# Attention with two heads stacked on partition halves as row tiles of TensorE, in a fused attention, ELU MLP and soft-MoE kernel

## What is computed

```python
def _attn_ref(q, k, v):
    B, H, S, D = q.shape                      # 4, 8, 1152, 64
    q_pool = q.reshape(B, H, S // 2, 2, D).mean(axis=3)
    scores = (1.0 / np.sqrt(D)) * np.matmul(q_pool, k.transpose(0, 1, 3, 2))
    scores = scores - np.max(scores, axis=-1, keepdims=True)
    attn = np.exp(scores)
    attn = attn / (np.sum(attn, axis=-1, keepdims=True) + 1e-09)
    return np.matmul(attn, v)

h = x @ w_in                                   # x: attention output, (2304, 512)
g = np.where(h > 0.0, h, np.exp(np.minimum(h, 0.0)) - 1.0)
x = g @ w_out
# soft MoE: logits = x @ phi; softmax over tokens gives the slots' inputs,
# two layers with a relu per expert, softmax over slots gives the outputs
```

## Time and profile before

| | |
|---|---|
| median of 3 runs | 1035.39 us (1034.98 to 1036.83) |
| profiled execution, span | 1034.5 us |
| granted TensorE clock, mean over the span | 0.979 of full speed |
| PE busy (matmul) | 959.7 us |
| DVE busy | 694.7 us |
| ACT busy | 499.0 us |
| POOL busy | 432.7 us |

### The profile page before, as it was taken

How to read it: one execution, slowest core, us unless ns; L and a number is a source line. 1 busy time by engine, 2 the same in 40 slices (tenths; PEclk the granted TensorE clock), 3 DMA queues, 4 the chain that set the end, 5 groups by cost and what they waited for, 6 DMA issues and landing times.

```text
span 1034.5 us, 17581 instructions
## 1 busy us (share of the span) xinstructions
PE 959.7 (93%) x6842; PEld 799.1 (77%) x6842; DVE 694.7 (67%) x1167; ACT 499.0 (48%) x1134; POOL 432.7 (42%) x155
## 2 busy tenths in 40 slices
PE   4799999999999999999979999999999999999795
PEld 2677667677667676767679999999999999999533
DVE  7769999999999999996577434444444444443423
ACT  3666666677666677665654323333323333232202
POOL 7887888988888888878900000000000000000000
PEclk9889999999999999999989999999999999999898
DMA  7621233322233332130061000020000000047995
GB/s 158 173 71 47 69 92 92 92 70 60 56 92 93 92 82 57 47 108 1 8 197 62 1 1 1 1 83 1 2 1 1 1 2 1 1 146 277 389 387 205
DMA packets 38946, 85.81 MB, mean 83 GB/s; under 512 B 3664, under 2 KB 11984, under 8 KB 38864
## 3 DMA queue, kind: packets, MB, share of 16 engines
q1 hardware_dynamic: 38864, 84.70, 27.1%
HBM read 79.97 MB, written 4.72 MB: 82 GB/s over the span
## 4 chain that ended last, share of the span: by engine, by line
PE 62%; DVE 32%; issue 3%; DMA 2%; ACT 1%; SPq 0%; DVEq 0%; ACTq 0%
DVE mx L921 8%; PE psum L530 7%; DVE kl L913 7%; PE psum L532 7%; PE psum L531 7%; PE psum L513 6%; PE psum L515 6%; PE psum L514 6%; DVE rinv L939 5%; DVE x L946 4%; PE psum L453 4%; DVE nm L932 3%; PE psum L454 3%; PE psum L421 3%; DVE q L903 2%
## 5 line engine op out<-in xcount | busy, mean ns | idle before, releaser
L1208 POOL TENSOR_TENSOR acc<-acc,pt 128x1152 f32<-128x1152 f32 x112 | 322.9, 2883 | 71.6 <-ACT pt L724 62.0
L724 ACT ACTIVATE pt<-psum 128x288 f32<-128x288 f32 x576 | 225.7, 412 | 153.4 <-PE psum L454 144.1
L921 DVE TENSOR_REDUCE mx<-psum 128x1 f32<-128x384 f32 x432 | 210.4, 546 | 30.8 <-PE psum L421 15.0
L453 PE MATMUL psum<-q,khh 128*128 128x288 f32 x576 | 181.0, 318 | 1.8 <-ACT pt L724 1.1
L454 PE MATMUL psum<-q,kl 66*128 66x288 f32 x576 | 170.8, 300 | 0.0
L530 PE MATMUL psum<-gh,W 128*128 128x288 f32 x512 | 158.4, 309 | 5.4 <-DVE gl L1002 5.4
L1080 DVE TENSOR_SCALAR g<-g 128x288 f32<-128x288 f32 x128 | 39.5, 309 | 175.1 <-ACT g L855 175.1
L532 PE MATMUL psum<-gh,W 128*128 128x288 f32 x512 | 151.6, 296 | 0.0
L513 PE MATMUL psum<-xh,W 128*128 128x288 f32 x512 | 151.6, 296 | 0.0
L514 PE MATMUL psum<-xl,W 128*128 128x288 f32 x512 | 151.4, 296 | 0.0
L531 PE MATMUL psum<-gl,W 128*128 128x288 f32 x512 | 151.2, 295 | 0.0
(11 more groups left out here) (113 smaller groups left out, 1393.5 us busy)
## 6 DMA issues: line engine op xcount, KB each, us to landing
ring<-in_w SPq DMA_DIRECT2D x32, 1024.0 KB, 7.5
kraw<-in_kT SPq DMA_DIRECT2D x64, 288.0 KB, 4.4
qraw<-in_qT SPq DMA_DIRECT2D x16, 576.0 KB, 5.7
vs<-in_v SPq DMA_DIRECT2D x16, 576.0 KB, 5.3
out<-ob SPq DMA_DIRECT2D x9, 512.0 KB, 4.9
wst<-in_w_in SPq DMA_DIRECT2D x16, 256.0 KB, 2.9
wst<-in_w_out SPq DMA_DIRECT2D x16, 256.0 KB, 3.6
sel<-in_selection SPq DMA_DIRECT2D x1, 96.0 KB, 8.3
```

The costliest lines, as they stand in the source:

```text
L453: mm(o, khh[:, p % NB, s, keys], q1[:, p % NB, a:a + HALF], start=True, stop=False)
L724: act.activation(pt[:, t % NPT, at:at + HALF], psum[:, T_BANKS[i % 3], 0:HALF], ACT.Exp, scale=SCALE).then_inc(s_exp, 1)
L921: dve.tensor_reduce(mx[:, p % 2, j, c:c + 1], r_bank(item)[:, 0:KC], AX.X, ALU.max).then_inc(s_red, 1)
L1208: pool.tensor_tensor(a, first, pt[:, t % NPT, :], ALU.add).then_inc(s_acc, 1)
```

## The change

The attention is written anew; the MLP and the mixture behind it stay as they are but for their PSUM banks and first waits.

- The two heads of a pair lie on partitions 0 to 63 and 64 to 127: one key load and one query load for both. Nothing is split into high and low parts for the second pass. Keys and queries are also cast to fp32r once (`khr`, `qhr`), for the maxima.
- A unit of the second pass is one key tile and one half of the queries for both heads (h counts the halves: h // 2 is the pair). It has four matmuls of 64 rows, two on each half of PE's rows: an fp32r one that puts down the negated maxima (`onesel` x `nmT`), and a plain fp32 one of keys and queries. The heads' scores go to two neighbouring banks, and one exponential reads both. There are two such slots, and the transposes of the maxima take a slot's turn too.
- The maxima come from 11 units a pair: eight of two row tiles of 512 keys, one of four pairs of 128 keys, one of two full matmuls of 512 and one of 128 keys, on a block-diagonal operand of the last 64 queries of both heads (`bdq`). Each unit but the last takes two banks of the ring of three.
- The softmax sums of one half (both heads) take one bank of that ring. DVE takes the reciprocal of 288 columns in PSUM, in place, and multiplies from there; the product's increment frees the bank.
- Value products come in two blocks per half: key tiles 5 to 8 of the half before ahead of key tile 5, and key tiles 0 to 4 at the end, followed by the sums of the half before.
- POOL adds up 576 columns at a time and has no other work. Six weight blocks of the MLP may be loaded and split before the attention ends (five before), in space that it doesn't use.

```diff
-    NPT = 6
+    NPT = 12
+    NU = 11
+    KC = 512
+    REM = SK - 2 * KC
+    X_AT = 5
...
+        ("pt", [P, NPT, 2, HALF], F32),
...
+        ("qraw", [P, 2, 2, SQ], F32),
...
+    WLEAD = W_EARLY
...
-    T_BANKS, R_BANKS, O_BANKS = (0, 1, 2), (3, 4, 5), (6, 7)
-    Y_BANKS, H_BANKS = (3, 4, 5, 6), (0, 1, 2, 7)
+    T_SLOTS, R_BANKS, O_BANK = ((0, 1), (2, 3)), (4, 5, 6), 7
+    Y_BANKS, H_BANKS = (4, 5, 6, 7), (0, 1, 2, 3)
...
+    def s_units(p, units):
+        return [("S", p, u) for u in units] if p < NP else []
+
+    def before_t(h, kt):
+
+        p = h // 2
+        if h == 0:
+            return s_units(1, {0: (0,), 1: (1,), 2: (2,), 4: (3,), 5: (5,), 7: (6,)}.get(kt, ()))
+        if h % 2 == 0:
+            return s_units(p + 1, {0: (2,), 2: (3,), 5: (5,), 7: (6,)}.get(kt, ()))
+        if kt == 7:
+            return s_units(p + 2, (0,))
+        return s_units(p + 1, {0: (7,), 2: (8,), 5: (10,)}.get(kt, ()))
+
+    def before_x(h):
+        return s_units(h // 2 + 1, (9,) if h % 2 else (4,))
+
+    def before_y(h):
+        return s_units(h // 2 + 2, (1,)) if h % 2 else []
+
+    def t_turns(h, kt):
+
+        rows = [("TR", h // 2 + 1)] if h % 2 and kt == 7 and h // 2 + 1 < NP else []
+        return rows + [("T", h, kt)]
+
+    r_items = s_units(0, range(NU))
+    t_items = [("TR", 0)]
+    for h in range(NH):
+        for kt in range(KT):
+            if kt == X_AT:
+                r_items += before_x(h)
+            r_items += before_t(h, kt)
+            t_items += t_turns(h, kt)
+        r_items += before_y(h)
+        if h:
+            r_items.append(("SUM", h - 1))
+    r_items.append(("SUM", NH - 1))
+    t_at = {item: n for n, item in enumerate(t_items)}
...
+    def banks_of(item):
+        return 1 if item[0] == "SUM" or item[2] == NU - 1 else 2
...
+    def r_bank(item, k=0):
+        n = use_at[item] + k
+        return psum[:, FIRST_BANKS[n % 6] if n < FIRST else R_BANKS[(n - FIRST) % 3], :]
+
+    def r_free(item):
+
+        n = use_at[item] + banks_of(item) - 1
+        if n < FIRST:
+            return max(n - 5, 0)
+        return n - 2 if n - FIRST >= 3 else FIRST
+
+    def t_free(item):
+        n = t_at[item]
+        if n < 2:
+            return None
+        old = t_items[n - 2]
+        return (s_trc, 3 * old[1] + 3) if old[0] == "TR" else (s_exp, KT * old[1] + old[2] + 1)
+
+    def t_slot(item):
+        return T_SLOTS[t_at[item] % 2]
+
+    def t_pair(item):
+        lo, hi = t_slot(item)
...
+        def load_k(p):
+            if p >= NB:
+                sp.wait_ge(s_Ta, 18 * (p - NB + 1))
+                sp.wait_ge(s_Tb, 18 * (p - NB + 1))
+            sp.dma_start(kraw[:, p % NB, :], kT[2 * p:2 * p + 2].rearrange("h d s -> (h d) s")).then_inc(d_k[p % NB], 16)
...
         load_q(0)
         load_k(0)
+        sp.dma_start(ident[:, :], eye).then_inc(d_eye, 16)
         load_k(1)
-        sp.dma_start(ident[:, :], eye).then_inc(d_eye, 16)
         load_q(1)
...
+            if r_free(item):
+                pe.wait_ge(s_red, r_free(item))
+            if item[0] == "SUM":
...
+                pe.wait_ge(s_acc, (KT - 1) * (h + 1))
...
+                for s in range(2):
+                    ins = mm(o[64 * s:64 * s + 64, 0:HALF], ones[:, :], acc[:, h % 2, s, :], start=True, stop=True)
+                ins.then_inc(s_Sf, 1)
+                return
+            p, u = item[1], item[2]
...
+            lo = r_bank(item)
+            if u == NU - 1:
+                mm(lo[:, 0:REM], bdq[:, b, :], khr[:, b, 2 * KC:], start=True, stop=True).then_inc(s_Sf, 1)
+                return
+            hi = r_bank(item, 1)
+            if u == NU - 2:
+                mm(lo, bdq[:, b, :], khr[:, b, 0:KC], start=True, stop=True).then_inc(s_Sf, 1)
+                mm(hi, bdq[:, b, :], khr[:, b, KC:2 * KC], start=True, stop=True).then_inc(s_Sf, 1)
+                return
+            if u < NU - 3:
+                j, c = u // 2, u % 2
+                pieces = [(slice(0, KC), slice(j * P, (j + 1) * P), slice(c * KC, (c + 1) * KC))]
+            else:
+                pieces = [(slice(j * REM, (j + 1) * REM), slice(j * P, (j + 1) * P), slice(2 * KC, SK)) for j in range(4)]
+            for to, queries, keys in pieces:
+                insA = mm(lo[:, to], qhr[0:64, b, queries], khr[0:64, b, keys], start=True, stop=True)
+                insB = mm(hi[:, to], qhr[64:P, b, queries], khr[64:P, b, keys], start=True, stop=True)
+            insA.then_inc(s_Sa, 1)
+            insB.then_inc(s_Sb, 1)
+
...
+            if t_free(item):
+                pe.wait_ge(*t_free(item))
+            pe.wait_ge(s_nm, 2 * p + 2)
...
+            for j in range(4):
+                nc.tensor.transpose(lo[0:65, j * P:(j + 1) * P], nm2[:, p % 2, j, :], ident[:, :])
+            nc.tensor.transpose(hi[0:65, 0:P], nm2[:, p % 2, 4, :], ident[:, :]).then_inc(s_TR, 1)
...
+            item = ("T", h, kt)
+            if t_free(item):
+                pe.wait_ge(*t_free(item))
...
+            lo, hi = (psum[:, k, 0:HALF] for k in t_slot(item))
+            keys = slice(kt * P, (kt + 1) * P)
+            q = slice(half * HALF, (half + 1) * HALF)
+            mm(lo, onesel[0:64, :], nmT[0:64, p % 2, q], start=True, stop=False)
+            mm(hi, onesel[64:P, :], nmT[64:P, p % 2, q], start=True, stop=False)
+            mm(lo, kraw[0:64, p % NB, keys], qs[0:64, p % NB, q], start=False, stop=True).then_inc(s_Ta, 1)
+            mm(hi, kraw[64:P, p % NB, keys], qs[64:P, p % NB, q], start=False, stop=True).then_inc(s_Tb, 1)
+
+        def times_v(h, kts):
...
+                    ins = mm(psum[64 * s:64 * s + 64, O_BANK, 0:HALF], vs[:, p % NB, s, kt * D:(kt + 1) * D],
+                             pt[:, i % NPT, s, :], start=(kt == 0), stop=(kt == KT - 1))
                 ins.then_inc(s_pv, 1)
...
+        pe.wait_ge(s_bd, 2)
+        for u in range(NU):
+            ring_item(("S", 0, u))
+        max_rows(0)
+        for h in range(NH):
+            for kt in range(KT):
+                if kt == X_AT:
+                    for item in before_x(h):
                         ring_item(item)
-                    done = due
-                if gi:
-                    times_v(p, gi - 1)
-                elif p:
-                    times_v(p - 1, G - 1)
-        times_v(NP - 1, G - 1)
+                    if h:
+                        times_v(h - 1, range(X_AT, KT))
+                for item in before_t(h, kt):
+                    ring_item(item)
+                if len(t_turns(h, kt)) == 2:
+                    max_rows(h // 2 + 1)
+                scores(h, kt)
+            for item in before_y(h):
+                ring_item(item)
+            if h == 0:
+                pe.wait_ge(s_one, 1)
+            times_v(h, range(X_AT))
+            if h:
+                ring_item(("SUM", h - 1))
+        times_v(NH - 1, range(X_AT, KT))
...
-                pe.wait_ge(s_o, NP)
-                pe.wait_ge(s_sum, 2 * NP)
+                pe.wait_ge(s_o, NH)
+                pe.wait_ge(s_red, uses)
...
                     if (c, f) == (0, 0):
-                        ring_item(("SUM", NP - 1, 0))
-                        ring_item(("SUM", NP - 1, 1))
+                        ring_item(("SUM", NH - 1))
...
+                act.wait_ge(s_Sf, n_f[("S", p - 2, NU - 1)] + 1)
+            act.copy(khr[:, p % 2, :], kraw[:, p % NB, :]).then_inc(s_khr, 1)
...
+            act.copy(qhr[:, b, :], q)
+            act.copy(bdq[0:64, b, 0:64], q[0:64, 4 * P:SQ])
+            act.copy(bdq[64:P, b, 64:P], q[64:P, 4 * P:SQ]).then_inc(s_qhr, 1)
...
+            lo, hi = (psum[:, k, :] for k in t_slot(("TR", p)))
+            act.wait_ge(s_TR, p + 1)
...
+            act.copy(nmT[0:65, b, 0:4 * P], lo[0:65, :]).then_inc(s_trc, 1)
+            act.copy(nmT[0:1, b, 4 * P:SQ], hi[0:1, 0:64]).then_inc(s_trc, 1)
+            act.copy(nmT[64:65, b, 4 * P:SQ], hi[64:65, 64:P]).then_inc(s_trc, 1)
+
+        def exps(h, kt):
+            i = KT * h + kt
...
+                old = i - NPT
                 act.wait_ge(s_pv, old + 1)
                 act.wait_ge(s_acc, (KT - 1) * (old // KT) + max(old % KT, 1))
...
+            act.activation(pt[:, i % NPT, :, :], t_pair(("T", h, kt))[:, :, 0:HALF], ACT.Exp, scale=SCALE)\
+               .then_inc(s_exp, 1)
+
+        def read_products(h):
+            p, half = h // 2, h % 2
+            act.wait_ge(s_pv, KT * (h + 1))
+            act.copy(x[:, 2 * (p // PB) + half, p % PB, :], psum[:, O_BANK, 0:HALF]).then_inc(s_o, 1)
...
+        keys_round(0)
+        queries_round(0)
+        keys_round(1)
+        queries_round(1)
+        read_rows_of_max(0)
+        for h in range(NH):
+            p = h // 2
+            for kt in range(KT):
+                if h % 2 and kt == 7 and p + 1 < NP:
+                    read_rows_of_max(p + 1)
+                exps(h, kt)
+                if h and kt == 6:
+                    read_products(h - 1)
+                if h % 2 == 0 and kt == 7 and p + 2 < NP:
```

(106 more changed lines are left out.)

478 lines of the change are left out of this document (127 added, 351 removed).

## The result

The kernel after takes 1053.18 us in the median of four runs (1052.67 to 1053.32), against 1035.49 for the kernel before (also the median of four): a ratio of 1.0164, 95% interval 1.015 to 1.0179. It is slower by 17.7 us. Forecast was 1032. The profiled execution has a span of 1050.9 us, 2.3 under the median, and stands for the runs.

What follows compares the result with a forecast made beforehand. Attention was taken as DVE-bound, PE close behind; DVE's relief is given back by more PE score work and a ring wait. Start +1.5, first pair -4.3, middle pairs -1.7, last +3, stage 1 -1.5: -3.0, 1032 us; eight in ten 992 to 1068.

Steps and rivals of the forecast that it cites:

- pair of 30.7 us: Attention, one pair of heads: even half 14.6 us, odd half to 16.1, together 30.7 us against 30.8 before.
- Score units, 0.61 us: Second pass on PE: one key tile and half, both heads, takes 0.13 + 0.48 = 0.61 us if row tiles run side by side.
- (b): Rival in PE's scores: units step in issue order, 0.73 us instead of 0.61; 1056 us; chance 0.25 including costlier tile changes and POOL-delayed product.
- (c): Rival in PE's scores: row tiles run one after the other, a unit takes 1.22 us; about 1180 us; chance 0.06.
- The ring wait, 1.77 us a half: Attention: PE stands 1.77 us each half until DVE's reciprocal and product free the sums' bank and its first reduction follows.
- rival (a): Attention: waits overlap better than laid out, a pair takes 28 to 30 us; 994 to 1022 us in all; chance 0.34.
- I take nothing: PE's changes between two row tiles and the whole array, five a pair, were priced at zero.
- The upper end: PE's changes between row tiles and whole array: at most 0.24 us each, five a pair, +1.2 us a pair, +17 in all.
- maximum units, put at 0.22: Maxima on PE: two row tiles of 512 keys together cost some 0.22 us, eight such units a pair.
- Stage 1 begins with 1.5 us less: MLP start: the first product of stage 2, waiting for DVE's last normalization, comes some 1.5 us earlier.
- Start +1.5: Kernel start: DVE's second query sum delays its reductions, so scores start near 30.3 us instead of 28.84, +1.5.
- Attention is DVE-bound by a little, with PE right behind: Kernel before, one pair: DVE busy 29.66 of 30.80 us, PE 28.22, so relieving DVE gains only down to PE's time and waits.

## Why the prediction was wrong

The size of the miss is 19.4 us of span (1050.9 against 1031.5) and 1.3 us between span and median. The 14 middle pairs gave 12.1 us of it, the first and last pair 2.5, the start of the MLP 8.0 and the rest 1.1; the start of the kernel gave 4.3 back. Two steps failed, then: the pair of 30.7 us, in its odd half, and the start of stage 1. By the forecast's own steps:

- **Score units, 0.61 us: right.** 0.62 measured. Rivals (b) and (c), units of 0.73 and of 1.22 us, are refuted. The time lands near (b)'s 1056, but not by its mechanism.
- **The ring wait, 1.77 us a half: right in kind, and nearly in size.** The forecast counted from the end of the stream; counted so it is 1.66 (246.13 + 0.24 to 248.03). The profile's 1.50 counts from the modelled end of the last matmul. The reciprocal took 1.97 us, and the product was never held up by POOL (0.46 in all 32). Copying the sums out gives 35 us, so it is the largest cost of the change that a run has shown, and without it the kernel would have been faster than before. This is why rival (a), a pair of 28 to 30 us, failed; with the sums copied out the pair is 29.3.
- **A pair of 30.7 us: too low by 0.85.** This step failed, 12 us over 14 pairs. The even half came out at 14.75 where the forecast had 14.6; 0.17 of that is its own addition (10.1, two scores of 0.61 and 0.35 of waits are 11.67, not 11.5). The odd half failed: 16.79 for 16.1, and 0.58 of the difference is there when the transposes start (11.03 us behind the end of the sums, forecast 10.45). "I take nothing" for the changes between row tiles and the whole array was wrong where fp32r matmuls are on both sides: 0.35 us a pair by the run without them, 5 of the 12 us. The upper end that I had named, 0.24 for each of five, was too high: there are four, and the two around the block-diagonal units cost 0.17 each. The rest is the likely price of the maximum units, put at 0.22. Behind the ring wait the odd half's four short matmul pairs take 263.28 - 262.78 = 0.50 (priced as 0.3), and between two score units a unit adds 0.86 - 0.37 = 0.49. In the even half the two scores behind such a unit then needed no wait, where 0.35 had been taken, which made up for it. No run of its own tested the price of these units.
- **Stage 1 begins with 1.5 us less: wrong, +6.5.** I looked at DVE's order and not at POOL's. The last half's additions still run when PE asks for their sums: 5.20 us of wait for 0.5 before, and matmuls at the lower clock behind it. Moving the sums two groups later made this stretch 5.0 us shorter, 3.2 in the span. DVE's product, which the forecast did watch, came no earlier: its stand is 5.26 us for 5.4 before.
- **Start +1.5: wrong, -2.8.** The queries' load came earlier than I had put it. First and last pair together came to 57.0 us, where I had 54.5.
- **"Attention is DVE-bound by a little, with PE right behind": not settled.** Freeing PE of 1.07 us a pair gave 0.35 and turned into waits for DVE, which fits. The run meant to free DVE of 2.4 us a pair took only a tenth of that off its busy time. The forecast didn't rest on a gain from DVE, so this cost it nothing.

The Trainium skill, TensorEngine Tiling, Key Properties, says that changing the tiling mode drains TensorE. The runs agree around the block-diagonal units, at 0.17 us a change. Ahead of the transposes they show no such cost, and behind them they can't tell.

The forecast gave 0.41 to slower and had 1053 inside its range of eight in ten, but that part of the range came from rival (b)'s units of 0.73, which did not occur: that the time fell inside it is luck. Its sum was made of small differences between large terms: 30.7 against 30.8 a pair. An error of 0.2 to 0.8 us in a term that comes 14 times decides the sign there.

## What to carry to other kernels

Before a long, slow operation reads PSUM in place, ask what else wants that bank. A 0.46 us copy out of a three-bank ring, with the reciprocal moved to a quiet place, was worth 35 us. When engines are this close, price every step that repeats, small matmuls and changes of tile mode too, and look at the last iteration's lagging engine where the next phase starts. Check in the trace that an edit meant to free an engine did free it: 29 us taken off one DVE line came back as 26.6 on two others. And look at the granted clock of every experiment: taking work away from TensorE made this kernel 24 us slower.
